# Chunk 0 of a delta-rule attention: quarter grams first, low weight parts on GpSimd, another order of ScalarE's work

## The reference, cut to what matters

```python
for t in range(S):                      # S = 768, per batch and head
    y[:, :, t] = einsum('bhd,bhde->bhe', q[:, :, t], state)
    v_old = einsum('bhde,bhd->bhe', state, kt)          # kt: k normalized
    state = state + bt * einsum('bhd,bhe->bhde', kt, vt - v_old)
x = y.transpose(0, 2, 1, 3).reshape(B * S, H * D)       # 3072 x 384
h = x @ w_in;  x = where(h >= 1, h, where(h <= -1, 0, (h + 1)**2 / 4)) @ w_out
h = x @ w_in2; x = maximum(h, 0)**2 @ w_out2            # d_ff = 2048
```

## Time and profile before

| what | us |
|---|---|
| median of three runs | 1006.88 |
| the profiled execution's own time | 1007.07 |
| its span, from the first to the last instruction | 1005.3 |
| TensorE busy | 987.7 |
| VectorE busy | 584.7 |
| ScalarE busy | 422.5 |
| GpSimd busy | 15.1 |
| mean granted TensorE clock, as a share of 2.4 GHz | 0.988 |

### The profile page before, as it was taken

One profiled execution on the slowest core, in us unless ns is written; L12 is line 12 of the kernel. 1 busy time (PEld: TensorE's weight loads), 2 busy tenths in 40 slices (PEclk: granted clock), 3 DMA queues, 4 the chain that ended last, 5 costly groups with the idle time before them and its releaser, 6 DMA issues.

```text
span 1005.3 us, 24704 instructions
## 1 busy us (share of the span) xinstructions
PE 987.7 (98%) x10462; PEld 807.2 (80%) x10462; DVE 584.7 (58%) x1468; ACT 422.5 (42%) x757; POOL 15.1 (1%) x30
## 2 busy tenths in 40 slices
PE   7899999999999999999999999999999999999998
PEld 6478788888888888888888888888888888888887
DVE  6669968776877687769545764333334334334332
ACT  4668544433443343443435554333333233333332
POOL 2200000000000000000000000000000000000000
PEclk7889999999999999999999999999999999999999
DMA  7233133003200320020002511001010010000000
GB/s 238 72 100 115 57 104 95 11 18 87 83 10 19 93 76 10 18 72 33 2 12 99 185 63 64 1 1 63 1 63 0 1 63 1 14 19 1 32 1 32
DMA packets 28413, 50.96 MB, mean 51 GB/s; under 512 B 2320, under 2 KB 15760, under 8 KB 28304
## 3 DMA queue, kind: packets, MB, share of 16 engines
q1 hardware_dynamic: 28304, 49.39, 15.3%
...
## 4 chain that ended last, share of the span: by engine, by line
PE 96%; ACT 1%; issue 1%; DMA 0%; DVE 0%; DVEq 0%; ACTq 0%; SPq 0%
PE psum L1140 40%; PE psum L1116 39%; PE psum L913 2%; PE psum L890 2%; PE psum L982 2%; PE psum L930 2%; PE psum L868 1%; PE psum L939 1%; PE psum L1067 1%; PE psum L1021 1%; PE psum L1029 1%; PE psum L1016 1%; PE psum L851 1%; PE psum L1044 1%; ACT ring L616 1%
## 5 line engine op out<-in xcount | busy, mean ns | idle before, releaser
L1140 PE MATMUL psum<-g_hi,w 128*128 128x512 f32 x1152 | 392.2, 395 | 0.0
L1116 PE MATMUL psum<-x_hi,w 128*128 128x512 f32 x1152 | 387.1, 390 | 0.0
L1406 DVE TENSOR_TENSOR g_lo<-act_g,g_hi 128x512 fp32r<-128x512 f32 x192 | 132.6, 691 | 214.6 <-ACT g_hi L752 214.6
L1140 PEld LDWEIGHTS psum<-g_hi,w 128*128 128x128 f32 x1152 | 216.1, 188 | 50.7 <-issue 2.0
L1116 PEld LDWEIGHTS psum<-x_hi,w 128*128 128x128 f32 x1152 | 216.2, 188 | 45.7 <-issue 0.2
L752 ACT ACTIVATE g_hi<-act_g 128x512 fp32r<-128x512 f32 x192 | 121.4, 632 | 273.8 <-PE psum L1140 239.8
L1140 PE MATMUL psum<-g_lo,w 128*128 128x512 f32 x576 | 224.6, 390 | 0.0
L1116 PE MATMUL psum<-x_lo,w 128*128 128x512 f32 x576 | 224.1, 389 | 0.0
L1400 DVE TENSOR_TENSOR act_g<-act_g 128x512 f32<-128x512 f32 x96 | 66.4, 692 | 112.9 <-ACT act_g L745 112.9
L1116 PEld LDWEIGHTS psum<-x_lo,w 128*128 128x128 f32 x576 | 108.1, 188 | 22.4 <-issue 0.2
L739 ACT ACTIVATE act_g<-act_g,half 128x512 f32<-128x512 f32 x87 | 62.9, 723 | 147.1 <-DVE act_g L1395 147.1
...
## 6 DMA issues: line engine op xcount, KB each, us to landing
...
```

What stands on the lines that cost most here:

```text
L1116: ins = pe.matmul(h_ps[n % 2][:, :], w_in_part(layer, f // GW, part)[:, kt, fs], x[:, kt, :], start=(kt == 0 and j == 0), stop=(kt == KT - ...
L1140: ins = pe.matmul(acc[kt][:, :], w_out_part(layer, f // GW, part)[:, f % GW, ds], g[n % 2][:, :], start=(f == 0 and j == 0), stop=(f == NF ...
L1406: dve.tensor_tensor(g_lo[n % 2][:, :], act_g[n % 2][:, :], g_hi[n % 2][:, :].bitcast(F32), ALU.subtract).then_inc(g_lo_ready, 1)
```

## The change

- The three warm-up products and their memset go.
- first_grams_of computes only the two 64x64 quarters on the diagonal of each head's gram (four products a pair of heads where there were two). The grams themselves are computed after all diagonal blocks are copied, by gram_of, in the layout of the later chunks (96x96), into the same banks.
- ScalarE's root comes ahead of its four gram copies.
- The low parts of weight groups 0, 1 and 2 are subtracted by GpSimd, in SBUF, behind the wait for xc: group 0 before the eight masks, group 1 and the x_inv memset behind them, then group 2. They count on a semaphore of their own, w_lo_early. TensorE's low_parts, ScalarE's low_out and VectorE's two subtractions go, with the waits on them (the first activations of ScalarE wait for w_lo_early 6).
- ScalarE scales all four block rows ahead of the solving and splits group 2 behind it.
- The fillers begin at inversion step 19 instead of 26, and the last is of 384 columns instead of 256.

```diff
-        def flat_part(g, part, out_part, half_of):
-
-            return weights[0][g][:, part, out_part, half_of * GW * DM // 2:(half_of + 1) * GW * DM // 2]
-
         def w_out_part(layer, g, part):
...
                     sp.wait_ge(w_hi_ready, split)
-                    sp.wait_ge(w_lo_ready, split)
+                    if g == 2 and not layer:
+                        sp.wait_ge(w_lo_early, split)
+                    else:
+                        sp.wait_ge(w_lo_ready, split - 2 * EARLY)
                 if layer and g == 0:
...
         def _(pool):
+            def low_parts(g):
+
+                for out_part in range(2):
+                    pool.wait_ge(ws_loaded[stage_of(0, g)[0]], 32 * stage_of(0, g)[1])
+                    pool.wait_ge(w_hi_ready, 2 * g + out_part + 1)
+                    part = w_out_part if out_part else w_in_part
+                    pool.tensor_tensor(part(0, g, LOW), staged(0, g)[out_part], part(0, g, HIGH).bitcast(F32),
+                                       ALU.subtract).then_inc(w_lo_early, 1)
+
             pool.memset(half[:, :], 0.5).then_inc(half_ready, 1)
...
                                base=0, pattern=[[1, P]], channel_multiplier=-1).then_inc(mask_ready, 1)
-            for square, value in ((eye, 1.0), (minus_eye, -1.0)):
-                pool.memset(square[:, :], value).then_inc(eye_ready, 1)
-            pool.wait_ge(eye_ready, 2)
-            for square in (eye, minus_eye):
-                pool.affine_select(out=square[:, :], in_=square[:, :], compare_op=ALU.is_equal, fill=0.0,
-                                   base=0, pattern=[[1, P]], channel_multiplier=-1).then_inc(eye_ready, 1)
+            pool.memset(eye[:, :], 1.0).then_inc(eye_ready, 1)
+            pool.wait_ge(eye_ready, 1)
+            pool.affine_select(out=eye[:, :], in_=eye[:, :], compare_op=ALU.is_equal, fill=0.0,
+                               base=0, pattern=[[1, P]], channel_multiplier=-1).then_inc(eye_ready, 1)
             pool.memset(u_sb[:, :, :], 0.0).then_inc(u_zero, 1)
...
             pool.wait_ge(xc_ready, 1)
+            low_parts(0)
             for m in range(B):
...
                                        pattern=[[0, HP], [1, P]], channel_multiplier=-1).then_inc(kq_ready, 1)
-            for n in range(NC - 1):
+            low_parts(1)
+            pool.memset(x_inv[:, :, :], 0.0).then_inc(x_zero, 1)
+            low_parts(2)
+            for n in range(1, NC - 1):
                 pool.wait_ge(xc_ready, n + 1)
...
-                if m < B:
-                    act.wait_ge(gd0_done, m + 1)
-                else:
-                    act.wait_ge(gram_done, m - B + 1)
+                act.wait_ge(gram_done, m + 1)
+                if m >= B:
                     act.wait_ge(first_s_done, HALVES * (NB - 1))
...
                 for hp in range(2):
-                    if m < B:
-                        blocks = g_ps(m)[hp][0:LATE, :].rearrange("p (h t) -> p h t", h=HP)[:, :, BLK:P]
-                    else:
-                        blocks = g_ps(m)[hp][0:LATE, 0:HP * LATE].rearrange("p (h t) -> p h t", h=HP)
+                    blocks = g_ps(m)[hp][0:LATE, 0:HP * LATE].rearrange("p (h t) -> p h t", h=HP)
                     act.activation(gram[m % B][0:LATE, hp * HP:(hp + 1) * HP, :], blocks, ACT.Copy).then_inc(gram_ready, 1)
...
-            def low_out(g, out_part):
-
-                for half_of in range(2):
-                    act.wait_ge(low_done, 4 * g + 2 * out_part + half_of + 1)
-                    act.activation(flat_part(g, LOW, out_part, half_of), low_ps[half_of][:, 0:GW * DM // 2], ACT.Copy
-                                   ).then_inc(w_lo_ready if half_of else low_half, 1)
-
             def square_part(n):
...
                     if n < 2:
-                        act.wait_ge(w_lo_ready, 2 * EARLY)
+                        act.wait_ge(w_lo_early, 2 * EARLY)
                         act.wait_ge(half_ready, 3)
...
             split_weights(0, 1, 1)
-            low_out(0, 0)
-            low_out(0, 1)
-            scaled_first(0, 0, H)
-            low_out(1, 0)
-            low_out(1, 1)
-            scaled_first(1, 0, H)
-            scaled_first(2, 0, H)
-            split_weights(0, 2, 0)
-            split_weights(0, 2, 1)
+            for k in range(NB):
+                scaled_first(k, 0, H)
             for k in range(NB):
...
                         solved_first(k, part, b)
-                    if k < 2:
-                        scaled_first(NB - 1, 2 * (HALVES * k + part), 2 * (HALVES * k + part) + 2)
                 if k == 1:
                     gain_root(1)
+            split_weights(0, 2, 0)
+            split_weights(0, 2, 1)
             for m in range(B):
...
             def first_grams_of(b):
+
                 pe.wait_ge(kt_loaded[b], 16)
                 for a in range(HP):
-                    for hp in range(2):
-                        k = kt_sb[hp * DP:hp * DP + D, b, a, :]
-                        ins = pe.matmul(g_ps(b)[hp][:, a * P:(a + 1) * P], k, k, start=True, stop=True)
+                    for quarter in range(2):
+                        for hp in range(2):
+                            rows = slice(quarter * DP, (quarter + 1) * DP)
+                            k = kt_sb[hp * DP:hp * DP + D, b, a, rows]
+                            ins = pe.matmul(g_ps(b)[hp][rows, a * P + quarter * DP:a * P + (quarter + 1) * DP], k, k,
+                                            start=True, stop=True)
                 ins.then_inc(gd0_done, 1)
...
                 n, b = divmod(m, B)
-                if n == 1 and b == 0:
+                if n == 0:
+                    pe.wait_ge(gd0_ready, NB * B)
+                elif n == 1 and b == 0:
                     pe.wait_ge(first_u_act, OWN * HALVES * NB)
...
                     pe.wait_ge(first_u_dve, (B - OWN) * HALVES * NB)
-                    pe.wait_ge(low_half, 4)
-                    pe.wait_ge(w_lo_ready, 4)
                 else:
...
-            def low_parts(g, out_part):
-
-                at, turn = stage_of(0, g)
-                pe.wait_ge(eye_ready, 4)
-                pe.wait_ge(ws_loaded[at], 32 * turn)
-                pe.wait_ge(w_hi_ready, 2 * g + out_part + 1)
-                pe.wait_ge(kq_plain, 2 * 2)
-                for half_of in range(2):
-                    wait(pe, w_lo_ready if half_of else low_half, 2 * g + out_part)
-                    out_ps = low_ps[half_of][:, 0:GW * DM // 2]
-                    whole_part = staged(0, g)[out_part].rearrange("p a c -> p (a c)")
-                    pe.matmul(out_ps, eye[:, :], whole_part[:, half_of * GW * DM // 2:(half_of + 1) * GW * DM // 2],
-                              start=True, stop=False)
-                    pe.matmul(out_ps, minus_eye[:, :], flat_part(g, HIGH, out_part, half_of).bitcast(F32),
-                              start=False, stop=True).then_inc(low_done, 1)
-
             def keep_busy(columns, out_ps):
+                pe.wait_ge(eye_ready, 2)
                 pe.wait_ge(gd_ready, 2)
...
+            def low_parts_ready(layer, g, out_part):
+                at = 2 * (layer * NG + g) + out_part + 1
+                if at > 2 * EARLY:
+                    pe.wait_ge(w_lo_ready, at - 2 * EARLY)
+                else:
+                    pe.wait_ge(w_lo_early, at)
+
             def first_product(n):
...
                     pe.wait_ge(w_hi_ready, 2 * (layer * NG + f // GW) + 1)
-                    pe.wait_ge(w_lo_ready, 2 * (layer * NG + f // GW) + 1)
+                    low_parts_ready(layer, f // GW, 0)
                 if n < 2:
...
                     pe.wait_ge(w_hi_ready, 2 * (layer * NG + f // GW) + 2)
-                    pe.wait_ge(w_lo_ready, 2 * (layer * NG + f // GW) + 2)
+                    low_parts_ready(layer, f // GW, 1)
                 pe.wait_ge(g_hi_ready, n + 1)
...
-            pe.wait_ge(tmp_zero, 1)
-            for _ in range(3):
-                pe.matmul(bank[7][:, 0:2 * P], tmp[:, 0:P], tmp[:, 0:2 * P], start=True, stop=True)
             for b in range(B):
                 first_grams_of(b)
+            for m in range(B):
+                gram_of(m)
             for hp in range(2):
...
                 keys_by_queries(m)
-            for g in range(2):
-                low_parts(g, 0)
-                low_parts(g, 1)
             pe.wait_ge(mask_ready, 2)
-            for j in range(26, BLK - 1):
+            for j in range(19, BLK - 1):
                 pe.wait_ge(inv_chain, inv_count(j))
...
             keep_busy(4 * P, bank[0])
-            keep_busy(2 * P, bank[0])
+            keep_busy(3 * P, bank[0])
             for part in range(HALVES):
...
-            dve.memset(tmp[:, 0:2 * P], 0.0).then_inc(tmp_zero, 1)
             for b in range(B):
...
             gains_turn(1)
-            split_weights(0, 2, 0)
             for m in range(B):
                 x_low_first(m)
-            split_weights(0, 2, 1)
             start_inverse(1)
```

17 lines of the change are left out of this document (5 added, 12 removed).

## The result

The changed kernel takes 999.78 us (median of four runs, 999.17 to 1000.42) against 1006.63 us for the kernel before beside it (four runs, 1006.14 to 1007.22): 6.85 us less, a ratio of 0.9932, 95% interval 0.9915 to 0.9949. It is faster, as forecast, by 0.7%, but the forecast was 995.3 us and its range ended at 998.9.

A forecast was written before the change was run, and what follows sets the result against it. A chain through several engines bounds the time ahead of 67.17 us, TensorE's instruction count the rest. 3.2 + 5.6 - 0.2 + 3.0 = 11.6 us off 1006.88 gives 995.3 us; own range 993.6 to 997.4, overall 993.4 to 998.9.

The forecast's parts named there:

- Earlier start: Inversion of the first chunk starts earlier through quarter grams: 3.2 us saved, bounds 0 and 3.6.
- Low parts off TensorE: Gap between the inversion's end and the first solve: 5.6 of 5.92 us saved, bounds 4.7 and 5.85.
- ScalarE's lateness: ScalarE's scalings of all four block rows ending late for the first solve's copies: 0.2 us charged, bounds 0 and 1.2.
- The moved load: Third weight group's load, released at 40.7 us by GpSimd's first two low parts: cost 0, 3 us of cover.
- The substitution chain: First solve to first outputs, without scalings between: 12.95 instead of 15.96 us, 3.0 saved, bounds 1.8 and 3.7.
- three rounds 10.2: Three solving rounds of copies, substitution, solve and handovers, 3.4 us each (3.2 to 3.8): 10.2 us.
- The end: Outputs to the dense part, 5.04 us set by TensorE: cost and gain 0, bounds 0 and +0.5.
- Rival 3: TensorE's clock stays at 1.2 GHz through the chain and into the outputs: 999.9 us, chance 8%.
- 1: First grams' quarters don't run side by side on TensorE, so the 3.2 us go: 998.5 us, chance 7%.
- 2: GpSimd and VectorE hinder each other in the chain, delaying four residual subtractions, 3.5 us: 998.8 us, chance 8%.
- 4: GpSimd's subtraction far dearer than its masks, holding ScalarE's first activations: 1008 us at 5 us each, chance 3%.
- 5: First solve still waits, for ScalarE's scalings or a late fourth query load: 997.7 us, chance 3%.

The follow-up runs named there:

- e4: Changed kernel with its first grams whole again (128x128) instead of quarters, the rest kept: 1000.26 us.
- e8: Changed kernel with the three warm-up products and their memset put back ahead of the grams: 999.39 us.
- e13: e12 with the filler behind the first solve of 512 columns instead of 256: 999.11 us.
- e11: e9 with the filler behind the first solve of 512 columns instead of 256: 1003.45 us.
- e15: The changed kernel once more, unaltered: 999.29 us.
- e5: Changed kernel with its twelve paced fillers replaced by one burst of 256 products of 32x32 without waits: 1001.43 us in one run.
- e3: Changed kernel with 640 filler columns more behind the first solve: 999.99 us.
- e9: e1 with the load of weight group 2 held back until the last solve, its splits behind the outputs' copies: 1003.58 us.
- e12: e1 with VectorE's five small gain instructions of chunk 1 moved behind the solving: 998.68 us.
- e7: e1 with all three fillers between the block rows of 512 columns instead of 256: 998.75 us.
- e1: Changed kernel with ScalarE's two high parts of weight group 0 moved ahead of its second copy of chunk 1's diagonals: 999.26 us.
- e10: e1 with GpSimd's low parts of group 0 ahead of its wait for xc, beside the inversion, releasing group 2's load earlier: 1000.13 us.

## Why the prediction was right in sign and too large

**Earlier start: right in its place, but hardly in the total.** The turn came at 9.29 us (predicted 8.7 to 9.4), and 2.92 + 0.13 us came off where 3.2 were forecast. But with the turn 1.46 us later again (e4) the total was only 0.5 us higher, less than can be told: most of what starts earlier here is lost to ScalarE's lateness, to the clock and to the hole. The quarters do run side by side: 128 records of the first grams end 4.2 us after the first began, waits for the loads included. The warm-up had indeed bought nothing (e8).

**Low parts off TensorE: right.** The gap is 0.15 us, 5.77 saved for 5.6. GpSimd's subtraction is 1.80 to 1.83 us long, as read off its masks. The estimate of 1.7 us, worked out in the prediction from a figure of the Trainium skill ("GPSIMD Engine Reference", "Performance versus the Vector engine"), is 0.1 us short of it.

**ScalarE's lateness: a term too small.** Charged 0.2 us, measured 1.1. The stall of TensorE ahead of keys by queries came back (2.95 us, and 2.98 in the earlier trace rows), and keys by queries began at 21.58 us, later than the 20.5 that I had given for this case. ScalarE's scalings ended at 39.19, later than the 38.7 "at the latest". The stall is a block of instructions too, behind record 156 instead of 150. I had written that ScalarE would be early "with the stall of TensorE gone", without a reason for it to go.

**The moved load: placed right, its cost open.** It was released at 40.94 us, 40.7 predicted, and its data were in time. But the cost of 0 counted only who waits for the data. Its traffic may also hold back the packet that brings TensorE's instructions. e13 suggests this with one packet; e11 has a hole of 0.80 us without the load, and e15 one of only 0.42 us with it. What the load costs wasn't separated, since moving it also moves the low parts behind it.

**The substitution chain: the step that failed.** Predicted 12.95 us with 0.2 on top, measured 16.21: 3.05 of the 4.65 us missing in the profiled execution. The term was "three rounds 10.2", at 3.4 us a round from the instructions that ScalarE and TensorE execute; they took 12.34. With the clock up three rounds take 10.01 us (e5) and 10.28 (e3), so the term is right for full clock and wrong for this chain. With the clock mostly at half and no hole (e8) they take 11.61; with it at half and the hole, 12.34. So about 1.3 us of the 2.1 are the clock and about 0.7 the hole, by differences between kernels that are not otherwise equal. The remaining 0.9 is the lateness above.

Two steps failed. The first is the bound of 3.8 us for a round, taken from a round of 3.77 us whose clock was low only in part: at half clock TensorE's own work fills 4.12 us (e8), and I had assumed "fewer holes" and nothing lost to the clock. The second is that a round was added up without the supply of instructions, which stops TensorE for 1.09 us in the third solve. The rows had shown it: the "issue" of 2.98 us, which I took for a stall that may go, is the same thing. As a steady rate, one block in 3.5 us, it would have cost only about 0.3 us over three rounds, an estimate; the rest of the hole is a block that came late, and why it did stays open.

**The end: also wrong, 1.62 us.** Rival 3, at 8%, was in part true. It priced this stretch at 2.5 us more with the clock at half; it was at half for 3.3 of the 6.66 us. Without a hole and at full clock it is 5.04 to 5.05 us (before, e4, e8). The profiled execution has no hole in its outputs; its four slow groups of 16 records took 3.38 us instead of 1.74, and these 1.6 us are the whole difference: the clock alone. The same kernel in another execution (e15), with the clock up, took 5.76 us: there 0.7 us are the supply, with the hole shown there. With wider fillers the clock fell later in three pairs of kernels (53.0 us in e3 and 43.3 in the changed kernel, 48.5 in e11 and 41.5 in e9, 45.3 in e13 and 42.2 in e12) and earlier in one (46.5 in e7, 47.6 in e1), and nothing was left of it in the total.

**Rivals.** 1 is false (the grams above). 2 is nearly nil in the changed kernel, 0.15 us, but true as soon as ScalarE is in time (e1) or GpSimd works beside the inversion (e10), and not through the residuals, which I had feared for, but through instructions with both inputs in SBUF. 3 gave 999.9 us, nearly the 999.78 measured, but by luck: its queued fillers (0.9 us) cost nothing and its outputs 1.6 instead of 2.5 us, while ScalarE's lateness and the hole were not in it. 4 did not happen, since 1.8 us was right. 5 did not happen as written: the first solve started 0.15 us behind xc, and ScalarE's lateness met the first copies instead.

**The range.** The 9.5 us at worst leave out two bounds that the prediction had itself, 1.2 us for ScalarE and 0.5 us at the end; with them its own range would have reached 999.1 us, still short of the measured 999.78. (At best, 13.15 us less is 993.7 us and not 993.6.)

What stays open: why the clock fell when it did, what the load adds, and why a block is not asked for sooner. The hole is not what made the clock fall in the changed kernel, where it fell 2.9 us ahead of it; in e15 and e12 too it fell first, and in e4 and e8 without any hole in the chain. Nor do the idle times ahead of it settle this: e1, e9 and e12 have the same ones in the first round (0.15 or 0.16, 0.5 and 0.23 us), and their clocks fell at 47.6, 41.5 and 42.2 us.
